# Attention of batches 1 to 3 placed between the steps of the first chunk, its heads in halves of the array

## What is computed

```
kv  = einsum('bhsd,bhse->bhde', k, v)          # 4 batches, 8 heads, 576 tokens, 64 wide
out = einsum('bhsd,bhde->bhse', q, kv)
x   = out / sqrt(mean(out*out, -1) + 1e-6) * g_norm       # to 2304 tokens x 512
h   = x @ w_in                                 # 512 x 2048
x   = (h * sigmoid(1.702 * h)) @ w_out         # 2048 x 512
h   = x @ w_in2
out = (max(h, 0) + log1p(exp(-abs(h)))) @ w_out2
```

## Time and profile before

| | us |
|---|---|
| median of 3 runs | 849.98 |
| lowest, highest | 847.45, 851.34 |
| the profiled execution | 849.25 |
| its span on the core | 847.4 |
| PE busy, PEld busy | 836.8, 710.1 |
| DVE, ACT, POOL busy | 428.9, 266.8, 185.5 |

### The profile page before, as it was taken

One profiled execution on the slowest core, in us unless ns is written; L12 is line 12 of the kernel. 1 busy time (PEld: TensorE's weight loads), 2 busy tenths in 40 slices (PEclk: granted clock), 3 DMA queues, 4 the chain that ended last, 5 costly groups with the idle time before them and its releaser, 6 DMA issues.

```text
span 847.4 us, 11420 instructions
## 1 busy us (share of the span) xinstructions
PE 836.8 (99%) x4136; PEld 710.1 (84%) x4136; DVE 428.9 (51%) x775; ACT 266.8 (31%) x505; POOL 185.5 (22%) x156
## 2 busy tenths in 40 slices
PE   7999999999999999999999999999999999999998
PEld 6987888998888888888888888888888888888897
DVE  3747434353334323444446754655565446555574
ACT  3665211111010211022234533433343333433343
POOL 0259410000000000004443532222212222222131
PEclk9999999999999999999999999999999999999999
DMA  9954300000000000002210100100010001000100
GB/s 299 347 202 149 124 26 1 1 1 1 1 1 0 0 0 0 0 0 94 90 64 26 50 1 0 50 0 0 0 50 0 0 0 50 0 0 0 50 2 26
DMA packets 13486, 36.12 MB, mean 43 GB/s; under 512 B 1552, under 2 KB 3216, under 8 KB 13456
## 3 DMA queue, kind: packets, MB, share of 16 engines
q1 hardware_dynamic: 12880, 35.39, 12.2%
q10 hardware_dynamic: 576, 0.33, 0.1%
HBM read 31.00 MB, written 4.72 MB: 42 GB/s over the span
## 4 chain that ended last, share of the span: by engine, by line
PE 96%; DMA 2%; DVE 1%; ACT 1%; issue 0%; DVEq 0%; ACTq 0%
PE ps L417 46%; PE ps L379 46%; PE ps L320 2%; PE ps L337 1%; DMA kv_in_sb<-k_v 1%; DMA tail_sb<-k_v 1%; PE ps L358 1%; PE ps L342 0%; DVE xs L608 0%; DVE gs L656 0%; PE ps L398 0%; ACT L553 0%; DVE xs L610 0%; DVE x_tok L601 0%; DVE rms L589 0%
## 5 line engine op out<-in xcount | busy, mean ns | idle before, releaser
L656 DVE CAST gs<-hid 128x512 fp32r<-128x512 f32 (+1 forms) x160 | 82.7, 517 | 275.9 <-PE ps L417 274.2
L379 PE MATMUL ps<-xs,w_shared 128*128 128x512 f32 (+1 forms) x960 | 210.1, 368 | 0.0
L379 PE MATMUL ps<-xs,w_own 128*128 128x512 f32 (+1 forms) x960 | 206.4, 368 | 0.1
L379 PEld LDWEIGHTS ps<-xs,w_shared 128*128 128x128 f32 x960 | 168.8, 188 | 30.6
L379 PEld LDWEIGHTS ps<-xs,w_own 128*128 128x128 f32 x960 | 167.8, 189 | 31.0 <-DVE xs L610 0.8
L294 POOL TENSOR_TENSOR stage<-stage 128x512 f32<-128x512 f32 (+1 forms) x80 | 94.6, 1182 | 290.5 <-DVE stage L638 290.5
L525 ACT ACTIVATE hid<-ps 128x512 f32<-128x512 f32 (+1 forms) x80 | 44.5, 556 | 260.9 <-PE ps L379 258.8
L658 DVE TENSOR_TENSOR gs<-hid,gs 128x512 fp32r<-128x512 f32 (+1 forms) x160 | 107.1, 669 | 5.6
L281 POOL TENSOR_TENSOR w_own<-stage,w_own 128x512 fp32r<-128x512 f32 x32 | 42.6, 1357 | 301.3 <-ACT w_own L455 301.3
L417 PE MATMUL ps<-gs,w_own 128*128 128x512 f32 (+1 forms) x480 | 105.2, 368 | 0.5 <-DVE gs L656 0.5
L529 ACT ACTIVATE stage<-ps 128x512 f32<-128x512 f32 (+1 forms) x80 | 44.5, 556 | 194.0 <-PE ps L379 175.7
(11 more groups left out here) (43 smaller groups left out, 407.0 us busy)
## 6 DMA issues: line engine op xcount, KB each, us to landing
stage<-moe_w SPq DMA_DIRECT2D x32, 512.0 KB, 3.3
kv_in_sb<-k_v SPq DMA_DIRECT2D x16, 512.0 KB, 8.4
q_sb<-q_t SPq DMA_DIRECT2D x16, 288.0 KB, 9.1
out<-xy SPq DMA_DIRECT2D x18, 256.0 KB, 2.2
tail_sb<-k_v SPq DMA_DIRECT2D x3, 256.0 KB, 10.3
tail_sb<-k_v ACTq DMA_DIRECT2D x1, 256.0 KB, 6.5
eye_sb<-eye ACTq DMA_DIRECT2D x1, 64.0 KB, 6.0
g_col<-g_norm ACTq DMA_DIRECT2D x2, 0.2 KB, 7.1
```

Source lines behind the costliest of these rows:

```text
L379: mm = nc.tensor.matmul(bank, w[:, W_IN, wp, cols], xs[:, xp, k, 0:width], start=(k == 0 and (wp, xp) == (HI, HI)), stop=(k == KT - 1 and ...
L656: nc.vector.tensor_copy(gs[:, HI, s, at:at + width], g).then_inc(g_hi_made, 1)
```

## The change

Only batch 0's attention stands ahead of chunk 0. The other three batches stand between chunk 0's blocks, at numbered places: place 2f is behind up f, place 2f+1 behind down f-3. At places 6, 11 and 16 PE makes the kv products of a whole batch, each in a 64-wide strip of bank 5; at twelve places up to 20 it makes one unit's raw output, all in banks 6 and 7; at places 22 to 27 it turns two pairs of units each. From step 2 on, all of chunk 0's up products go to bank 4 alone. ACT and DVE have the same places in their queues. For the late batches ACT takes the roots of a batch at once, with a table load ahead and behind, and DVE first reads the raw output out of its banks unscaled, and scales the batch later in place.

The two heads of a unit are no longer one product with unused blocks: the kv product is two of 64x64 in column halves of the array, the raw output two of 128x64 in row halves, each half into a bank of its own. ACT then copies all of kv. Unit and q buffers shrink to one batch, `w_shared` from 8 to 5 steps, and SP's order is written out by hand.

```diff
-KV_BANK, RAW_EVEN, RAW_ODD, TURN_EVEN, TURN_ODD = 0, 1, 2, 4, 5
+RAW_FIRST = {0: 4, 1: 6, 2: 0, 3: 2}
+LATE_KV, LATE_RAW = 5, 6
+LATE_TURN = (5, 6, 7)
...
+        KV_AT = {6: 1, 11: 2, 16: 3}
...
+        ROOT_AT = {5: 1, 8: 2, 10: 3}
+        SCALE_AT = {6: 1, 9: 2, 11: 3}
...
+        def hid_bank(f, first=False):
+            if first:
+                return {0: 5, 1: 1}.get(f, HID_BANK)
...
+                    for h in range(2):
+                        r = slice(h * D, (h + 1) * D)
+                        mm = nc.tensor.matmul(ps[r, bank, first:first + D], tile[:, 0, r], tile[:, 1, r],
+                                              start=(t == 0), stop=(t == MAIN))
...
+            def late_kv(batch):
+                if batch == 1:
+                    pe.wait_ge(hid_read, HID_BANKS + 1)
+                else:
+                    pe.wait_ge(kv_copied, PAIRS * batch)
+                for u in range(batch * PAIRS, (batch + 1) * PAIRS):
+                    kv_product(u)
...
+                    pe.wait_ge(kv_copied, (u // PAIRS + 1) * PAIRS)
+                    if u == PAIRS:
+                        pe.wait_ge(x_made, 2)
+                    else:
+                        pe.wait_ge(raw_read, u - PAIRS)
+                o = raw(u)
                 for t in range(MAIN):
+                    for h in range(2):
+                        r = slice(h * D, (h + 1) * D)
+                        main, _ = q_tokens(u, p)
+                        mm = nc.tensor.matmul(o[:, h, t * D:(t + 1) * D], main[r, t * P:(t + 1) * P],
+                                              kv_sb[r, p, :], start=True, stop=True)
...
+            def first_chunk():
...
+                up(0, 0, 0, CHUNK, 0, range(0, 2), first=True)
+                turn(2)
+                up(0, 0, 0, CHUNK, 0, range(2, 3), first=True)
+                turn(3)
+                up(0, 0, 0, CHUNK, 0, range(3, 4), first=True)
+                for f in range(1, FT + DOWN_LAG):
+                    if f == DOWN_LAG:
+                        pe.wait_ge(x_made, PAIRS)
+                        pe.wait_ge(hid_read, HID_BANKS + 2)
+                    if f < FT:
+                        if f >= 3:
+                            pe.wait_ge(hid_read, HID_BANKS + f)
+                        up(f, 0, 0, CHUNK, 0, first=True)
+                        attention(2 * f)
+                    if f >= DOWN_LAG:
+                        down(f - DOWN_LAG, 0, 0, CHUNK, 0)
+                        attention(2 * f + 1)
...
+                    if first:
+                        attention(2 * f)
+                        if f + W_AHEAD < FT - 1:
+                            split_high(f + W_AHEAD)
+                        attention(2 * f + 1)
...
+            W_AHEAD = 3
...
+            for u in range(PAIRS):
                 sum_squares(u)
                 scale(u)
+                if u >= 1:
+                    dve.wait_ge(x_made, u)
+                    split_x(0, 0, CHUNK, [u - 1])
+            dve.wait_ge(x_made, PAIRS)
+            split_x(0, 0, CHUNK, [PAIRS - 1])
```

More of the change, by code:

```diff
@@ new lines, in attention @@
+            def attention(place):
+                if place in KV_AT:
+                    copy_kv(KV_AT[place] * PAIRS, PAIRS)
+                if place in RAW_AT:
+                    square(RAW_AT[place])
+                if place in TURN_AT:
+                    gain(2 * TURN_AT[place])
+                    gain(2 * TURN_AT[place] + 1)
+            act.dma_start(tail_sb[0:TAIL].rearrange("p u a n -> p u (a n)"),
+                          k_v[0:PAIRS, MAIN * P:S].rearrange("u p n -> p u n")).then_inc(tail_in, 16)
@@ L497, in _ @@
             act.wait_ge(acc_copied, ACC_BANKS)
+            act.wait_ge(consts_in, 48)
             copy_kv(0)
-            act.wait_ge(consts_in, 48)
-            for u in range(UNITS + TURN_LAG):
-                if u + 1 < UNITS:
-                    copy_kv(u + 1)
-                if u < UNITS:
-                    square(u)
-                if u >= TURN_LAG:
-                    gain(u - TURN_LAG)
-                if u < UNITS:
-                    root(u)
+            copy_kv(1)
+            square(0)
+            copy_kv(2)
+            root(0)
+            square(1)
+            copy_kv(3)
+            root(1)
+            square(2)
+            gain(0)
+            root(2)
+            square(3)
+            gain(1)
+            root(3)
+            split_high(0)
+            gain(2)
+            gain(3)
+            nc.scalar.preload_act_table_set("sigmoid_and_others")
+            split_high(1)
+            split_high(2)
             def copy_acc(ci, j, dst, src, last=False):
@@ L605, in split_x, with attention @@
+            def attention(place):
+                if place in RAW_AT:
+                    read_raw(RAW_AT[place])
+                    sum_squares(RAW_AT[place])
             def split_x(ci, tok0, width, tiles=range(KT)):
```

432 lines of the change are left out of this document (255 added, 177 removed).

## The result

| | before | after |
|---|---|---|
| median of 4 runs, us | 849.93 | 884.43 |
| lowest, highest | 847.45, 851.34 | 883.5, 886.31 |
| profiled execution, its span | 849.25, 847.4 | 884.16, 882.4 |
| chunk 1's first matmul | 142.57 | 177.53 |

The ratio is 1.0415, with a 95% interval of 1.0398 to 1.0431: 34.5 us slower, where 16.0 were forecast. The time is in the range (848 to 886), at its upper end. From chunk 1's first matmul to the end of the span it is 704.9 us against 704.8 before, so all of it was lost ahead of chunk 1, and the 18.5 us by which the forecast of 159.0 fell short have to be found there.

What follows compares the result with a forecast made beforehand. It took PE to bound the kernel, with memory also binding attention; 30.0 + 0.7 + 84.3 + 27.5 + 15.0 + 1.5 = 159.0 us to chunk 1, against 142.6, gave a forecast of 866 us, range 848 to 886.

Steps and rivals of the forecast that it cites:

- (6): After a wait PE restarts slowly: 1.5 us, put behind the 6 us wait alone, bounds 0 and 6.
- (1): Batch 0's attention alone, up to chunk 0's last x tile, with a chain over three engines: 30.0 us.
- (2): Chunk 0's own up and down products, unchanged: 0.7 + 84.3 us.
- (3): Attention of batches 1 to 3 between chunk 0's blocks, at 45 ns a record plus transposes: 27.5 us.
- (4): New PE waits between chunk 0's steps, from load order, ACT's roundings and the shared up bank: 15.0 us.
- (5): Paired turns, fewer buffers, roundings on ACT: nothing more; batch scales up to 4 us a batch if DVE loses cover.
- (a): Rival: both array halves run side by side, waits as forecast; late attention 19.3 us, total 861 us; chance 17 in 100.
- (b): Rival: side by side and weights don't queue behind kv loads; faster than before, 844.7 us; with its neighbours 14 in 100.
- (c): Rival: records stay at 111 ns, 896 us (6 in 100); milder form, only the raw output's, 882 us (12).
- (d): Rival: records at 55 ns, heads not parallel in time, plus 3 us of mode-change drains; 874 us; chance 10 in 100.
- What could be won: PE's start before the change: some 11 us of holes and slow records that ideal overlap could win, plus some products.

Runs made afterwards that it cites:

- e7: Kernel after with weights 6 to 10 ahead of the kv loads, step 2's up product in its own bank, first kv copied before ACT's constants wait: 866.80 us.
- e5: Kernel after with five unread fp32 products of 128x512 ahead of and between the first kv products: 880.20 us.
- e9: e7 plus unread matmuls at the start, ahead of each of the last three x tiles and ahead of unit 11: 859.08 us.
- e3: Kernel after with weights 6 to 8 loaded ahead of the tail, kv and q loads that stood before them: 875.50 us.
- e4: Kernel after with 11, 15 and 30 unread matmuls filling the three long waits, order unchanged: 881.99 us.
- e11: e9 with whole products instead of halves: 860.97 us.
- e6: Kernel before with four unread fp32 products of 128x512 in its first waits: 849.11 us, ratio 0.9998.
- e12: Kernel before with the kv product alone in column halves, the raw output whole: 848.64 us, ratio 0.9987.
- e10: e2 with four unread fp32 products of 128x512 in its first waits: median 849.13 us; six of eleven runs 848 to 849, the others 856 to 873.
- e2: Kernel before, order untouched, with the heads in column halves (kv) and row halves (raw output): 866.39 us, ratio 1.0211.

## Why the prediction was right, and where it was wrong

The direction was right, and so was the place: all of the change lies ahead of chunk 1. The size, 16.0 us of 34.5, was less than half. The step that failed is the price of the slow clock: (6) put 1.5 us on it where 8.0 were measured, and (1) put nothing on it, where it cost 4.6 of the 6.8 us that (1) was short. A third term, blocks that take longer beside attention, was left out of the sum and is 4.2 us. The steps:

**(1) Batch 0 to the last x tile, 30.0: wrong, 36.8.** The chain of 3.5 us a tile over DVE is there, but the tiles stand 4.56 and 5.00 us apart. Two things were missed. The first kv copy stands behind ACT's wait for the constants (unit 0's raw output starts at 10.77, in e7 without that wait at 8.71); the last x tile of e7 is 2.2 us earlier. The rest is the clock: products, transposes and the chain through them ran at half pace up to 39 us, and with unread matmuls at the start (e5) the last x tile is 4.6 us earlier. I had read from the earlier trace rows that slow records end by 13 us, and took this for a time, where it depends on what PE does. With both repaired and the waits filled (e9) the tile starts at 29.57, so the chain itself was sized right: 11.2 us for three tiles from a first one at 18.40, where 10.5 from 19.5 were forecast.

**(2) Chunk 0's own products, 85.0:** as forecast, once what stands beside them is counted apart.

**(3) Late attention, 27.5: right in sum (28.1), not in its parts.** I took 45 ns for every record. The kv records take 29 ns, side by side, and the raw records 65 ns, more than half of a whole one: a mean of 47. Whole, the two heads' product is 2 records of 111 ns; in column halves it is 4 of 29, 1.9 times as fast, and in row halves 4 of 65, a sixth slower. The Trainium skill ("TensorEngine Tiling (Array Packing)", Theoretical Speedup) promises up to twice the speed for a dimension of 64. The column halves bear it out. The row halves, whose stationary operand still has 128 columns, don't. (The weight loads of the earlier trace rows were busy for 9.7 to 10.0 of 10 us, not for 9.9 at the least.)

**(4) New waits, 15.0: right in kind, and in sum (15.2) partly by luck.** Unit 8 waited 7.6 (6.0 forecast), unit 5 4.3 (3.3), up 3 2.9 (2.3), up 1 0.4 (1.2); the 1.2 of unit 7 and the 1 of small ones didn't come. The three long waits are 3.2 us above their forecast and the small ones 3.0 below theirs. Nothing came later, and e3 shows the mechanism. The waits for the x tiles were 5.3 where 7 to 9 were forecast, since the slow products ahead of them filled part.

**(5) Nothing more:** true of the kernel after, where no wait answers to the batch scales. Once their cover is gone, in e7, they cost 3.3 us, 2.1 of them by the two stretched operations.

**(6) Slow restart, 1.5 with bounds 0 and 6: wrong, 8.0.** I counted one wait; the clock fell behind all three, and behind each of them up to two pieces of work paid. Of the 8.0, 2.2 stand behind the waits for the x tiles. The sum of waits was right and the price of a wait was not: behind waits of 2.9, 4.3 and 7.6 us stand 1.3, 2.5 and 2.0 us of slow work, so the price doesn't grow with the wait. e4 bears the cause out, not the whole size: it got back 2.4 of the 5.8.

**The rule that I left out of the sum.** I quoted from the Trainium skill ("TensorEngine Tiling (Array Packing)", Tiling Modes) that a change of mode drains the engine, worked out 0 to 4.8 us, and added nothing. The trace has a cost of that kind: a block with a half-array product behind it takes 2.95 against 2.72, at 15 places, some 3.5 us, and blocks beside fp32 transposes 2.84. But beside whole fp32 products, with nothing in halves, it is 2.82 already (e11). So 0.13 us at each place, 2 us in all, is the most that drains can have cost, and that this part is a drain isn't shown.

Together, (1), (3), (4), (6) and the longer blocks: 6.8 + 0.6 + 0.2 + 6.5 + 4.2 = 18.3 of the missing 18.5 us.

**The rivals.** (a), side by side, is true of kv alone. (b), faster, is out: the loads queue (ACT's 13.70), and with them out of the way e3 and e7 are still 2 to 3% slower. (c), its milder form of 882 us, is closest in time and right in that the raw output is slow, but with 65 ns for its 111; the number agrees by accident. (d), with drains, had the right extra term at 3 us, where the blocks show 4.2. None had the clock as its mechanism. What would have pointed to it is in the prediction's own text: "the first records took double", priced at 1.5.

**What could be won** was put at 11 us of holes and slow records. e6 shows that almost nothing of the latter was to be had: chunk 0 starts 0.5 us earlier, and the waits for loads take the rest. In e12, with kv products at half the price, it starts 2.15 us earlier of up to 7.6 expected from PE's queue.

What stays open: why row halves don't bring the clock up while column halves beside whole products do, and why they hold it in some runs of e10 and not in others. e12 has both kinds of product in turn, so column halves with nothing whole beside them weren't tried, nor row halves beside whole kv products.

## What to carry to other kernels

Work that is moved out of a dense phase to fill another has to bring its own cover: here the first batch's chain over three engines lost the cover of the later batches, and that alone is 8 us in e9, which with every wait filled still ends 9.5 us above the kernel before. Price a wait of PE with what follows it at half the clock: here waits of 2.5 to 7.6 us were followed by 1 to 2.5 us of slow work. Look, too, whether the work ahead lets the clock come up at all. Splitting heads makes a unit's kv product 0.58 us instead of 1.12 in column halves and its raw output longer in row halves, and no kernel here was measurably faster for it, in an attention phase that memory bounds as well.

## What was not expected of the hardware

- With the raw output in row halves and kv in column halves PE stays at half pace until 35 us in e2, with PE busy for 10.0 of each 10 us from 10 us on, against 12 to 13 us in the kernel before and in e12. In e10, too, PE was busy throughout: the clock read 0.50 to 0.52 from 20 to 70 us in such work, behind waits of 0.38, 0.50 and 1.08 us; e12, with whole raw outputs, went through six waits of 0.2 to 0.8 us without a fall. A clock that was up did hold in halves in six of e10's eleven runs.
- A scale of 128x512 on DVE took 1.74 us instead of 0.69, and one of 128x128 1.38 instead of 0.28, while POOL made a weight's low half (e7, and the same in e9).
- The column of the granted clock reads 1.00 up to 48 us in the kernel after, though the pace is half up to 39, and 0.50 in the same kind of slow stretch later. In the start of these traces it can't be relied on.
- A block of 12 split matmuls takes 2.72 us among its like, 2.84 beside fp32 transposes, 2.82 beside whole fp32 products and 2.95 beside halves.
